# Another order of the token blocks, and one sum moved to TensorE, in a kernel of windowed attention and a two-layer MLP

## The reference

```python
def _attn_ref(x, weight_gen):           # x (4, 4096, 192); weight_gen (4, 4096, 8, 7)
    w = weight_gen - np.max(weight_gen, axis=-1, keepdims=True)
    w = np.exp(w)
    w = w / (np.sum(w, axis=-1, keepdims=True) + 1e-09)
    x_pad = np.concatenate([np.zeros((B, K - 1, D)), x], axis=1)
    idx = np.arange(S)[:, None] + np.arange(K)[None, :]
    x_unf = x_pad[:, idx, :].reshape(B, S, K, H, D // H)
    return np.einsum('bshk,bskhg->bshg', w, x_unf).reshape(B, S, D)

def _moe_ref(x, w_in, w_out, s, b):     # x (16384, 192); w_in (192, 2048); w_out (2048, 192)
    r = np.maximum(x @ w_in, 0.0)
    return (s * (r * r) + b) @ w_out
```

## Time and profile before

| | |
|---|---|
| median of 3 runs | 1140.21 us (1140.19 to 1141.2) |
| profiled execution | 1141.12 us |
| its span, first to last instruction | 1139.4 us |
| granted TensorE clock, mean | 0.996 |
| busy: TensorE | 1129.6 us, 99%, 12956 matmuls |
| busy: VectorE | 918.6 us, 81% |
| busy: ScalarE | 721.5 us, 63% |
| busy: GpSimd | 123.1 us, 11% |
| DMA, mean | 94 GB/s, 106.73 MB |

### The profile page before, as it was taken

The page is one execution under the profiler, slowest core; times in us unless marked ns, Lnnn a source line. Parts: engine busy times, 40 slices in busy tenths (PEclk is TensorE's granted clock), DMA queues, the critical chain, the costliest instruction groups (busy, mean ns, idle before and its releaser), DMA issues.

```text
span 1139.4 us, 31575 instructions
## 1 busy us (share of the span) xinstructions
PE 1129.6 (99%) x12956; PEld 1030.3 (90%) x12956; DVE 918.6 (81%) x1106; ACT 721.5 (63%) x746; POOL 123.1 (11%) x79
## 2 busy tenths in 40 slices
PE   8999999999999999999999999999999999999998
PEld 6999999999999999999999999999999999999997
DVE  8999887788877788877888777888778887778834
ACT  6776665566566666665665666566656666666663
POOL 2100111100111101111001111011110011110111
PEclk8999999999999999999999999999999999999999
DMA  9512334333244343343332442433433334424121
GB/s 254 92 54 61 86 91 118 87 94 102 76 108 117 69 112 80 89 117 87 95 93 80 113 117 65 116 77 92 117 81 100 84 86 116 117 65 116 35 59 29
DMA packets 97417, 106.73 MB, mean 94 GB/s; under 512 B 7187, under 2 KB 77730, under 8 KB 97390
## 3 DMA queue, kind: packets, MB, share of 16 engines
q1 hardware_dynamic: 94437, 103.61, 34.9%
q0 software_dynamic: 2512, 2.26, 1.3%
q10 hardware_dynamic: 440, 0.47, 0.2%
HBM read 70.63 MB, written 35.39 MB: 93 GB/s over the span
## 4 chain that ended last, share of the span: by engine, by line
PE 98%; DVE 1%; DMA 0%; ACT 0%; issue 0%; SPq 0%; DVEq 0%; ACTq 0%
PE hp L1033 47%; PE op L1071 35%; PE op L1078 16%; DMA x_in<-in_x 0%; PE op L949 0%; PE op L955 0%; SPq L231 0%; DVE scratch L810 0%; DVE scratch L806 0%; DVE g_lo L762 0%; ACT scratch L464 0%; ACT g_hi L471 0%; DVE wo L725 0%; DVE scratch L780 0%; ACT xT1s L438 0%
## 5 line engine op out<-in xcount | busy, mean ns | idle before, releaser
L1071 PE MATMUL op<-wo,g_hi 64*128 64x384 f32 x4096 | 594.3, 356 | 1.2 <-DVE g_lo L762 1.1
L1078 PE MATMUL op<-wo,g_lo 64*128 64x192 f32 x4096 | 514.3, 247 | 0.0
L460 ACT ACTIVATE scratch<-hp 128x1024 f32<-128x1024 f32 x254 | 255.7, 1019 | 376.3 <-PE hp L1033 374.3
L762 DVE TENSOR_TENSOR g_lo<-scratch,g_hi 128x1024 fp32r<-128x1024 f32 x255 | 324.1, 1272 | 186.5 <-ACT g_hi L471 182.3
L1078 PEld LDWEIGHTS op<-wo,g_lo 64*128 64x128 f32 x4096 | 392.5, 188 | 5.3
L1071 PEld LDWEIGHTS op<-wo,g_hi 64*128 64x128 f32 x4096 | 385.3, 184 | 7.2 <-issue 1.5
L1033 PE MATMUL hp<-xT1s,w_hi 64*128 64x512 f32 x2048 | 320.3, 390 | 0.5 <-ACT xT1s L438 0.3
L464 ACT ACTIVATE scratch<-scratch 128x1024 f32<-128x1024 f32 x255 | 269.9, 1059 | 6.0
L1033 PEld LDWEIGHTS hp<-xT1s,w_hi 64*128 64x128 f32 x2048 | 183.0, 185 | 33.9 <-issue 0.6
L1033 PE MATMUL hp<-xT1s,w_lo 64*128 64x512 f32 x1024 | 202.4, 391 | 0.0
L675 DVE TENSOR_TENSOR tap<-x_in,w_soft 128x768 f32<-128x768 f32 x186 | 177.5, 955 | 3.2
(11 more groups left out here) (74 smaller groups left out, 281.1 us busy)
## 6 DMA issues: line engine op xcount, KB each, us to landing
x_in<-in_x SPq DMA_DIRECT2D x30, 960.0 KB, 4.9
x_bounce<-x_parts SPq DMA_DIRECT2D x116, 192.0 KB, 3.4
xT1s<-x_bounce SPq DMA_DIRECT2D x29, 512.0 KB, 3.8
xT2s<-x_bounce SPq DMA_DIRECT2D x58, 256.0 KB, 4.9
out<-scratch SPq DMA_DIRECT2D x124, 96.0 KB, 1.8
w_in<-in_weight_gen SPq DMA_DIRECT2D x32, 112.0 KB, 2.1
wo_raw<-in_moe_w_out SPq DMA_DIRECT2D x4, 384.0 KB, 7.4
wo_sums<-in_moe_w_out POOLq DMA_DIRECT2D x4, 384.0 KB, 6.9
```

What stands on the lines that cost most here:

```text
L460: nc.scalar.activation(r[:, b, :], hp[:, PAIR * b:PAIR * (b + 1), :], ACT.Relu).then_inc(relu_done, 1)
L762: nc.vector.tensor_tensor(g_lo[:, buf, tiles, :], pair, g_hi[:, buf, tiles, :].bitcast(F32), ALU.subtract).then_inc(g_lo_ready, 1)
L1071: nc.tensor.matmul(op[:, t, 0:2 * D], g_hi[rows[h], g % 2, j, t * P:(t + 1) * P], wo[rows[h], k, :, :].rearrange("p a d -> p (a d)"), star ...
L1078: mm = nc.tensor.matmul(op[:, t, 0:D], g_lo[rows[h], g % 2, j, t * P:(t + 1) * P], wo[rows[h], k, 0, :], start=False, stop=(k == FT - 1 an ...
```

## The change

- The blocks are taken in the order 2, 3, ..., 31, 0, 1 (AHEAD = 2). Steps 0 to 29 load and store block i + 2; the last two steps do blocks 0 and 1.
- The first step's x comes in three DMAs over all 128 rows, all on SP's queue: the last 4 tokens, the 3 before them, the first 3. Second step's x is one `load_x`. There is no halo and no zeroing at the start.
- The halo is loaded near the end, by `load_edge_x`, for steps 30 and 31: for each of 4 batches one DMA of 31 rows and one that copies zeros from a new tile `zeros` into the batch's first row, then a wait of SP for all eight, then the rest of x.
- In the first step ScalarE's half product belongs to tap 1 instead of tap 0, so tap 0 is a whole product on VectorE.
- In step 1 VectorE leaves out the last addition. TensorE transposes both `acc` and the last product, accumulating, in `sum_second_attn` (32 matmuls where there were 12). The parts of xT2 are then taken from one block instead of two. The counts of `sum_ready` are one lower from there on.
- TensorE's loop begins at instruction slot 24 of a fetch block (`head_slot`), with padding ahead of it that is jumped over.

```diff
-            load_w(0)
-            load_first_x(0)
-            load_halo(sp, 0, first_halves)
+            load_w(AHEAD)
+            load_part_of_x(PAD, STEP, x_loaded[0])
+            load_part_of_x(PAD // 2, PAD // 2, x_first_loaded[0])
+            load_part_of_x(0, PAD // 2, x_first_loaded[1])
             load_w1(0)
             load_wo(0)
             load_wo(1)
             sp.wait_ge(w_shifted, 1)
-            load_w(1)
+            load_w(1 + AHEAD)
             load_w1(1)
             load_w1(2)
-            load_first_x(1)
-            load_halo(sp, 1, ((1, 120), (121, 7)))
+            load_x(1 + AHEAD, 1)
...
+            def load_edge_x(block):
+                missing = PAD - STEP * block
+                sp.wait_ge(zeros_ready, 1)
+                for q in range(B):
+                    a = q * batch_rows
+                    sp.dma_start(x_in[a + 1:a + batch_rows, block, 0:missing, :],
+                                 x_rows[a:a + batch_rows - 1, (TOK - missing) * row:TOK * row]).then_inc(x_edge_loaded[block], FETCH)
+                    sp.dma_start(x_in[a:a + 1, block, 0:missing, :].rearrange("p t d -> p (t d)"),
+                                 zeros[q:q + 1, 0:missing * row]).then_inc(x_edge_loaded[block], FETCH)
+                sp.wait_ge(x_edge_loaded[block], 2 * B * FETCH)
+                sp.dma_start(x_in[:, block, missing:, :], x_rows[:, 0:STEP * (block + 1) * row]).then_inc(x_loaded[block], FETCH)
...
-            loads(STEPS - 4, 0)
+            edge_loads(STEPS - 4, 0)
             bounce(STEPS - 3, 1)
             store(STEPS - 5)
-            loads(STEPS - 3, 1)
+            edge_loads(STEPS - 3, 1)
             bounce(STEPS - 2, 0)
             store(STEPS - 4)
             bounce(STEPS - 1, 1)
             store(STEPS - 3)
-            store(STEPS - 2)
+            store(STEPS - 2, 0)
...
-                products(K - 1, 0, STEP).then_inc(tap_ready, 1)
-                products(K - 2, 1, STEP - 1)
-                dve.wait_ge(x_halo_loaded[0], 2 * B * FETCH)
-                dve.wait_ge(pool_zeroed, PAIR)
-                dve.wait_ge(dve_zeroed, B - PAIR)
-                products(K - 2, 0, 1).then_inc(tap_ready, 1)
-                for k in reversed(range(1, K - 2)):
-                    products(k, 0, STEP).then_inc(tap_ready, 1)
-                products(0, 0, STEP - ACT_TOK).then_inc(tap_ready, 1)
+                for k in reversed(range(K)):
+                    if k == K - 2:
+                        dve.wait_ge(x_first_loaded[0], FETCH)
+                    if k == PAD // 2 - 1:
+                        dve.wait_ge(x_first_loaded[1], FETCH)
+                    products(k, 0, STEP - ACT_TOK if k == ACT_TAP else STEP).then_inc(tap_ready, 1)
...
-                if K - 1 in ks:
+                if K - 1 in ks and not first:
                     add_tap(i, K - 1, by_pe)
...
+            def sum_second_attn():
+                for n, part in enumerate((acc[:, :, :], tap[:, (K - 1) % 2, :, :])):
+                    for t in range(STEP):
+                        for h in range(2):
+                            last_a = nc.tensor.matmul(hp[:, h, t * D2:(t + 1) * D2], part[rows[h], t, 0:P], ident[rows[h], rows[h]],
+                                                      start=n == 0 and t == 0, stop=n == 1 and t == STEP - 1, is_transpose=True)
+                last_a.then_inc(t_ready, 1)
+                for n, part in enumerate((acc[:, :, :], tap[:, (K - 1) % 2, :, :])):
+                    for t in range(STEP):
+                        for h in range(2):
+                            last_b = nc.tensor.matmul(hp[:, 2 + h, t * D2:(t + 1) * D2], part[rows[h], t, D - P:D], ident[rows[h], rows[h]],
+                                                      start=n == 0 and t == 0, stop=n == 1 and t == STEP - 1, is_transpose=True)
+                last_b.then_inc(t_ready, 1)
...
                         if transposes_here and j == GROUP - 1:
-                            pe.wait_ge(sum_ready, (K - 1) * (i + 1))
+                            pe.wait_ge(sum_ready, sums_through(i + 1))
+                            if first:
+                                pe.wait_ge(tap_ready, K * (i + 2))
...
-            with pe.Fori(1, STEPS // 2 - 1) as j:
+            with nc.Fori(1, STEPS // 2 - 1, engines=bass.OrderedEngineSet([pe.engine]), head_slot={pe.engine: HEAD_SLOT}) as j:
```

More of the change, by code:

```diff
@@ L84, in mix_and_mlp @@
         ones = sb("ones", [P, P])
+        zeros = sb("zeros", [B, PAD * D])
         ident = sb("ident", [P, P])
@@ L224, in by_token @@
             return rows.rearrange("p (u e h c) -> p u e h c", u=STEP // 2, e=2, h=2)[:, :, e, :, :]
[L226 to L232, removed]
         def store_last(queue, n, t):
@@ L236, in store_last, with sums_through @@
                             out_sb[t * Q:(t + 1) * Q, n * PAIR:(n + 1) * PAIR, :]).then_inc(last_stored, FETCH)
+        def sums_through(i):
+            return (K - 1) * i - (1 if i > 0 else 0)
         batch_rows = S // TOK
[L239 to L246, removed]
         @block.sync
@@ L252, in _, with load_w, load_x, load_part_of_x @@
             wcol = STEP * H * K
-            def load_w(i):
-                sp.dma_start(w_in[:, :, :], w_rows[:, bass.ds(i * wcol, wcol)]).then_inc(w_loaded, FETCH)
-            def load_x(i, parity):
+            def load_w(block):
+                sp.dma_start(w_in[:, :, :], w_rows[:, bass.ds(block * wcol, wcol)]).then_inc(w_loaded, FETCH)
+            def load_x(block, parity):
                 sp.dma_start(x_in[:, parity, :, :],
-                             x_rows[:, bass.ds((i * STEP - PAD) * row, (STEP + PAD) * row)]
+                             x_rows[:, bass.ds((block * STEP - PAD) * row, (STEP + PAD) * row)]
                              ).then_inc(x_loaded[parity], FETCH)
-            def load_first_x(i):
-                before = PAD - STEP * i
-                sp.dma_start(x_in[:, i, before:, :], x_rows[:, 0:(STEP * (i + 1)) * row]).then_inc(x_loaded[i], FETCH)
+            def load_part_of_x(first, n, loaded):
+                sp.dma_start(x_in[:, 0, first:first + n, :],
+                             x_rows[:, (AHEAD * STEP - PAD + first) * row:(AHEAD * STEP - PAD + first + n) * row]).then_inc(loaded, FETCH)
+            def load_edge_x(block):
[9 more added lines that the diff above has]
+                sp.dma_start(x_in[:, block, missing:, :], x_rows[:, 0:STEP * (block + 1) * row]).then_inc(x_loaded[block], FETCH)
             def load_w1(g):
@@ L326, in loads, with edge_loads @@
                 sp.wait_ge(w_shifted, i + 2)
-                load_w(i + 2)
+                load_w(i + 2 + AHEAD)
                 sp.wait_ge(tap_ready, K * (i + 1))
-                load_x(i + 2, parity)
+                load_x(i + 2 + AHEAD, parity)
+            def edge_loads(i, block):
+                sp.wait_ge(w_shifted, i + 2)
+                load_w(block)
+                sp.wait_ge(tap_ready, K * (i + 1))
+                load_edge_x(block)
             loads(0, 0)
@@ L374, in _ @@
                                     base=0, pattern=[[-1, P]], channel_multiplier=1).then_inc(ident_ready, 1)
-            pool.wait_ge(ident_ready, 1)
+            nc.gpsimd.memset(zeros[:, :], 0.0).then_inc(zeros_ready, 1)
             def sum_wo(c):
@@ L664, in taps @@
                         dve.wait_ge(x_loaded[parity], x_count)
-                        if halo:
-                            dve.wait_ge(x_halo_loaded[1], 2 * FETCH)
-                            dve.wait_ge(pool_zeroed, PAIR + B)
+                        if first:
+                            pass
                         elif by_pe or after_pe:
@@ L831, in first_step @@
                 lo_of_w1(2)
-                taps(1, 1, range(0, 2), FETCH, halo=True, by_pe=True)
+                taps(1, 1, range(0, 2), FETCH, first=True, by_pe=True)
                 split_g(0, 2, True)
@@ L836, in first_step @@
                 lo_of_w1(3)
-                taps(1, 1, range(2, 5), FETCH, halo=True, by_pe=True)
+                taps(1, 1, range(2, 5), FETCH, first=True, by_pe=True)
                 split_g(0, 4)
                 split_g(0, 5, rounded=True)
-                taps(1, 1, range(5, K), FETCH, halo=True, by_pe=True)
+                taps(1, 1, range(5, K), FETCH, first=True, by_pe=True)
                 lo_of_wo(3, wo_lo3_ready)
@@ L901, in step @@
                     taps(i + 2, 1 - parity, range(0, 2), x_count)
-            for q in range(PAIR, B):
-                zero_batch_start(nc.vector, 0, q).then_inc(dve_zeroed, 1)
             shift_weights(0)
@@ L1082, in second_product @@
                         mm.then_inc(bank_left, 1)
-                    if transposes_here:
+                    if transposes_here and first:
+                        sum_second_attn()
+                    elif transposes_here:
                         transpose_attn_a()
```

69 lines of the change are left out of this document (33 added, 36 removed).

## The result

| | median | lowest to highest | runs |
|---|---|---|---|
| before | 1140.2 us | 1139.92 to 1141.2 | 9 |
| changed | 1144.13 us | 1141.84 to 1144.63 | 9 |

The ratio is 1.003, 95% interval 1.002 to 1.004. The change is slower by 3.9 us, 0.34%: on the side of the rivals, and 0.3 us above the upper end of the range. The profiled execution took 1143.53 us, span 1141.8.

A forecast was written before the change was run, and what follows sets the result against it. TensorE, holding 98% of the chain that ended last, was taken as the bound. -1.65 - 0.75 + 3.1 = +0.7 us took the profiled 1141.12 to 1141.8, median 1140.9; range 1137.5 to 1143.8 us.

The forecast's parts named there:

- The likeliest case: Whole kernel: one engine moves the 31-row copies at 26.4 GB/s, clock kept; 1140.9 us, chance 0.54.
- The other side: the new wait lowers the clock: Rival at step 29: TensorE's waits drop its clock to 0.50, losing 1.7 us more; 1142.6 us, chance 0.24.
- The start: Before the first product: fewer memsets and full-height x copies start it at 13.2 instead of 14.84; -1.65 us, bounds -2.3, -0.75.
- The second x: Step 1's x: VectorE's dropped addition brings g_lo earlier, so TensorE waits less; -0.75 us, bounds -0.95 and +0.1.
- The loop's slot: TensorE's loop: one added jump over padding, code not loaded anew each pass; zero, upper bound 0.9 us.
- The blocks moved last: SP's queue before step 29: 31-row copies on one engine delay x_bounce beyond its slack; +3.1 us, bounds 0 and +16.5.
- The case that the copies are spread: Rival near the end: several engines share the 31-row copies, nothing is late; 1137.8 us, chance 0.16.
- The rule on transposes: TensorE's start: if transposes do not count as busy for the clock, the start gains only -0.75 us instead of -1.65.

The follow-up runs named there:

- split16: The changed kernel with each batch's copy of 31 rows split into copies of 16 and 15 rows; 1138.32 us, 0.9984 of before.
- second_on_dve: split16 with the last addition of the second x back on VectorE and 12 transposes instead of 32; 1139.12 us, 0.9991 of before.
- slot200: split16 with TensorE's loop beginning at instruction slot 200 instead of 24; 1183.84 us, 1.0381 of before.
- two_single: The changed kernel with two of the four batches copied as 16 and 15 rows, two still as 31; 1138.28 us, 0.9981 of before.
- wait_behind: The changed kernel, 31-row copies kept, with SP's wait for them and the rest of x moved behind step 29's x_bounce; 1144.23 us, 1.0039 of before.
- slow_start: split16 with the first six tokens of the first x in eight 16-row copies on two queues, no memsets; 1141.15 us, 1.0007 of before.

## Why the prediction was right or wrong

The likeliest case said 1140.9 and no change; the result was 1144.13. What failed is the choice between two cases: the forecast kept the clock at step 29, and the sum has no term for it. The case that came is the rival "*The other side: the new wait lowers the clock*", which had 0.24: it named the place (step 29), the way (3.1 us of waits in two parts, at xT1 and xT2) and 1142.6.

- **The start, -1.65 (bounds -2.3, -0.75).** In the profiled executions -2.24, at the bound for a clock that stays full, which it did. In medians less: split16 is 2.0 below before, of which second_on_dve gives 0.8 to the second term, so about -1.2. The difference is probably in the executions of before: the one in the earlier trace rows had the clock at 0.50 from 8.3 to 15, a mean clock of 0.996, and took 1141.12, 0.9 above its median; of the 75 executions of before beside the experiments only two have a mean of 0.997 or less. The prediction took its terms from the traced execution and applied them to the median. The steps by themselves stood: max at 2.91 (said 3.0), products from 5.62 to 11.4 (5.7 to 11.4), no wait for x.
- **The second x, -0.75.** 0.8 in medians. TensorE's hole before the half product is gone, and the 32 transposes ran from 43.9 to 44.9, one microsecond, 0.84 said.
- **The loop's slot, 0.** Right for this slot: 21 packets, no hole. But the prediction looked only at the jump and not at where the pass ends, which is what slot200 shows to matter: 45.5 us.
- **The blocks moved last, +3.1.** 3.4 in the profile, 3.5 in the run of 1141.84. One engine, 27 GB/s (26.4 said), the rest of x issued 24.7 us after the first edge copy (24 said). The case that the copies are spread is ruled out by the share of 0.07. The Trainium skill (DMA: Bandwidth & Descriptors, Why a DMA increments its semaphore by 16 and not by 1), by which a copy of 31 rows goes over one engine, agrees with this trace.
- **What was left out: the clock, +1.4 to +2.8.** I weighed against it that the pause in the earlier trace rows was followed by short transposes and this one by dense products. That was no reason: what the two falls have in common is how little TensorE had done ahead of them (1.53 us of 3.4 in the earlier trace rows, 0.99 of 4.0 here). By the prediction's own numbers TensorE would do 0.7 us of work in 3.8 at step 29, less than in the earlier trace rows, so the fall was the likelier case and should have been in the sum, at 1142.6. The remaining 1.5 us are three small misses: 0.4 at the start and the second x together (-2.0 in medians where I said -2.4), 0.4 in the waits (3.5 for 3.1), and 0.6 in the clock (2.3 in the median for 1.7). The 1.7 came from a low stretch of 3.4 us, for which the prediction had no row: in the earlier trace rows the clock is at 0.50 over two rows, 6.6 us. The traced execution of the change has 3.4 us, but it is the one with the mean clock of 0.999. Six of the others have 0.997 or 0.996, which is 7 to 9 us at half the clock (my estimate: the missing 0.003 or 0.004 of 1142 us, times two), up to about 2 of them after the last product as in split16. So in most executions the low stretch was probably nearer to the length in the earlier trace rows. None of them is traced, and the times don't follow the mean clock one by one (1143.21 us has 0.997), so this stays an estimate.
- **The rule on transposes.** By the Trainium skill (TensorE: Matmul & The Clock Gate, Part 4: PE-mode transpose) transposes don't count as busy. In the changed kernel TensorE did nothing else from 6.7 to 12.2 and the granted clock stayed at 1.00: the trace again disagrees with the page, as the earlier trace rows did.

The parts, in medians: -1.2 (start) -0.8 (second x) +3.5 (waits) +2.3 (clock) = +3.8, against +3.9. The start and the clock are what is left after the others are taken off, so the agreement is no check of them; the check is the profiled sum above, +2.4.

The best kernel here is the change with no copy of 31 rows that matters, split16 at 1138.32 us, or two_single, the same within the measurement: 0.9984 [0.9975, 0.9993] of before and 0.5% below the change.

## What to carry to other kernels

Look at the number of rows of each DMA, not at its bytes: here four copies of 31 rows, on one engine, held the queue for 24.7 us where the same bytes in copies of 16 and 15 took 8, with all that is around them, and a copy that seems hidden by tens of microseconds can still hold an in-order queue past the slack of what stands behind it. Work out that slack for each thing queued behind, and when a wait of TensorE remains, price it twice, once for its length and once for the clock that it may cost. Here waits of 3.4 us (in two parts) and of 4.15 us cost the clock, one of 1.13 at the same place did not.

Moving a wait back in the queue is no cure while the slow transfer stays: what is let past still comes late, and what is moved back is late for its own reader (wait_behind).

## What the runs showed of the hardware that was not expected

- TensorE's loop is sensitive to where its first instruction lies: 1648 instructions a pass from slot 24 or 128 run without any reload, from slot 200 with 9 packets of 16 KB and a hole of 2.0 to 2.6 us at each back edge, 45.5 us in all. Without a fixed slot the traced execution loaded nine packets anew once, for 6.6 us with the clock's fall behind it; by their times the other eleven did not.
- One DMA engine alone moves 27 GB/s with rows of 4608 bytes; behind four such copies the issue of a small copy took 5.01 us instead of 0.6.
- While copies of 15 and 16 rows ran, four on each of two queues, the core moved 189 GB/s with all engines busy (190 in slow_start), and 306 with copies of 128 rows.
- The granted clock stayed at 1.00 through 5.5 us in which TensorE did only transposes.
